# A transformer block on one core: the order of the mixer's groups between the attention heads

## The reference

```
scores = q @ k.T / 8                      # 4 batches x 8 heads, 576 positions, 64 features a head
attn   = softmax(scores, block-causal)    # block of 64
x      = attn @ v                         # heads put side by side: 576 x 512

h = relu(x @ w_in)                        # 512 -> 1024
u, v = h[:, :512], h[:, 512:]
v_n = (v - mean(v)) / sqrt(var(v) + 1e-6)
v_s = w_spatial @ v_n + b_spatial[:, None]  # mixes positions, 576 x 576
x = (u * v_s) @ w_out                     # 512 -> 512

xn  = (x - mean(x)) / sqrt(var(x) + 1e-6) * g_ln
out = x + relu(xn @ w_ch1) @ w_ch2        # 512 -> 2048 -> 512
```

## Time and profile before

| what | us |
|---|---|
| median of three runs | 867.6 |
| lowest, highest | 867.1, 869.02 |
| the profiled execution, time | 869.89 |
| the profiled execution, span from first to last instruction | 868.1 |
| TensorE busy in it | 836.6 (96%) |
| VectorE, ScalarE, GpSimd busy | 348.9, 290.5, 203.2 |
| mean granted clock of TensorE, as a share of full speed | 0.988 |

### The profile page before, as it was taken

One profiled execution on the slowest core, in us unless ns is written; L12 is line 12 of the kernel. 1 busy time (PEld: TensorE's weight loads), 2 busy tenths in 40 slices (PEclk: granted clock), 3 DMA queues, 4 the chain that ended last, 5 costly groups with the idle time before them and its releaser, 6 DMA issues.

```text
span 868.1 us, 13430 instructions
## 1 busy us (share of the span) xinstructions
PE 836.6 (96%) x5064; PEld 709.4 (82%) x5064; DVE 348.9 (40%) x774; ACT 290.5 (33%) x784; POOL 203.2 (23%) x289
## 2 busy tenths in 40 slices
PE   7989999999999999998989999999999999999998
PEld 4766787768877688777969999999999999999997
DVE  5876644365443664417464312213222123122111
ACT  5865654355543554424344111111111111111110
POOL 4874646243341442503341000000000000000000
PEclk9999999999999999999989999999999999999999
DMA  6551321221212221016343003003003002001000
GB/s 212 163 174 42 112 81 42 77 86 58 69 43 76 80 65 42 2 54 194 98 147 114 1 1 109 1 0 109 0 0 109 0 0 90 18 0 43 30 1 36
DMA packets 37681, 56.02 MB, mean 65 GB/s; under 512 B 2749, under 2 KB 20157, under 8 KB 37630
## 3 DMA queue, kind: packets, MB, share of 16 engines
q1 hardware_dynamic: 37630, 55.34, 19.5%
HBM read 45.90 MB, written 9.44 MB: 64 GB/s over the span
## 4 chain that ended last, share of the span: by engine, by line
PE 51%; issue 4%; POOL 1%; DVE 1%; ACT 0%; POOLq 0%; ACTq 0%; DVEq 0%
PE psum L1017 17%; PE psum L1016 17%; PE psum L1015 17%; PE psum L1083 1%; POOL rstd L494 0%; POOL unit_raw L536 0%; DVE mix_buf L820 0%; POOL x_r L503 0%; DVE units_r L864 0%; DVE y_res L921 0%; DVE units_r L866 0%; POOL probs L483 0%; DVE mix_buf L810 0%; ACT x_r L616 0%; ACT units_r L682 0%
## 5 line engine op out<-in xcount | busy, mean ns | idle before, releaser
L908 DVE SCALAR_TENSOR_TENSOR h_r<-psum,h_r 128x384 fp32r<-128x384 f32 x96 | 53.5, 557 | 287.0 <-ACT h_r L709 287.0
L709 ACT ACTIVATE h_r<-psum 128x384 fp32r<-128x384 f32 x96 | 47.2, 492 | 340.5 <-PE psum L1017 340.5
L1015 PE MATMUL psum<-xn_r,units_r 128*128 128x384 f32 x384 | 129.6, 337 | 0.0
L1017 PE MATMUL psum<-xn_r,units_r 128*128 128x384 f32 x384 | 129.3, 337 | 0.0
L1016 PE MATMUL psum<-xn_r,units_r 128*128 128x384 f32 x384 | 128.9, 336 | 0.0
L483 POOL TENSOR_SCALAR probs<-probs,row_inv 128x512 f32<-128x512 f32 (+4 forms) x160 | 95.6, 612 | 139.2 <-DVE row_inv L759 139.2
L569 ACT ACTIVATE probs<-psum,neg_max 128x512 f32<-128x512 f32 (+4 forms) x160 | 89.1, 564 | 95.9 <-DVE neg_max L746 95.7
L746 DVE TENSOR_REDUCE neg_max<-psum 128x1 f32<-128x512 f32 (+4 forms) x160 | 77.6, 535 | 92.5 <-PE psum L938 92.3
L1017 PE MATMUL psum<-units_r,h_r 128*128 128x512 f32 x288 | 113.7, 395 | 0.0
L1016 PE MATMUL psum<-units_r,h_r 128*128 128x512 f32 x288 | 113.5, 394 | 0.0
L1015 PE MATMUL psum<-units_r,h_r 128*128 128x512 f32 x288 | 111.9, 389 | 0.0
(11 more groups left out here) (101 smaller groups left out, 1477.5 us busy)
## 6 DMA issues: line engine op xcount, KB each, us to landing
qk_raw<-qk SPq DMA_DIRECT2D x32, 576.0 KB, 4.0
unit_raw<-w_ch SPq DMA_DIRECT2D x32, 256.0 KB, 3.1
y_norm<-y_scratch SPq DMA_DIRECT2D x6, 768.0 KB, 5.8
y_res<-y_scratch SPq DMA_DIRECT2D x6, 768.0 KB, 4.6
out<-y_res SPq DMA_DIRECT2D x18, 256.0 KB, 2.1
v_raw<-vN SPq DMA_DIRECT2D x16, 256.0 KB, 3.0
y_scratch<-mix_buf SPq DMA_DIRECT2D x16, 256.0 KB, 2.0
w_raw<-w_in SPq DMA_DIRECT2D x8, 256.0 KB, 4.8
```

The lines of the kernel that those rows point to most:

```text
L709: act.activation(h_hi[:, f % HR, :], h_bank[:, f % 2, 0:CHUNK], ACT.Relu).then_inc(h_hi_done, 1)
L908: dve.scalar_tensor_tensor(h_lo[:, f % HR, :], h_bank[:, f % 2, 0:CHUNK], 0.0, h_hi[:, f % HR, :].bitcast(F32), ALU.max, ALU.subtract).the ...
L1015: pe.matmul(dst, a_hi, b_hi, start=start, stop=False)
L1017: return pe.matmul(dst, a_lo, b_hi, start=False, stop=stop)
```

## The change

Six things are done at once.

- `GROUP_STEPS`: the groups of a batch go to the steps of its eight heads as 3, 3, 4, 4, 4, 4, 2, 2, where they went as 3, 3, 3, 4, 3, 3, 3, 4.
- The list is moved by one place (`groups_at`): the first place of a batch's heads now holds w4 of the batch before. The last place after all heads (`groups_at(HEADS, 0)`) is used for w4 of the last batch but one, with its copy and its store.
- The s groups go half by half: d = i % 4, h = i // 4. So w0 waits for the low parts of the first four s groups only, and w2 for all eight.
- ScalarE reads a group at the start of steps 0 and 2 (ahead of the exponentials and copies) and at the end of steps 1 and 3; it did so at the end of every step. `split_at` is three steps after the group, not two; VectorE does the split ahead of the normalisation and the statistics.
- `tail_mixer` is gone. In the tail ScalarE reads u groups ahead of the split of the v group two before, an s group's parts are made in its own turn and ahead of the unit, VectorE does the split of g-2, the normalisation of g-1 and the statistics of g; the store of a w group is issued ahead of the unit loads.
- The transposes of the first chunk come ahead of w3, the `xn_tile` splits after w2.

```diff
-        GROUP_STEPS = [[0, 2, 3], [0, 2, 3], [0, 2, 3], [0, 1, 2, 3], [0, 2, 3], [0, 2, 3], [0, 2, 3], [0, 1, 2, 3]]
+        GROUP_STEPS = [[0, 2, 3], [0, 2, 3], [0, 1, 2, 3], [0, 1, 2, 3], [0, 1, 2, 3], [0, 1, 2, 3], [0, 2], [0, 2]]
-            return [(b, sum(len(r) for r in GROUP_STEPS[:i]) + GROUP_STEPS[i].index(step))]
+            at = GROUPS * b + sum(len(r) for r in GROUP_STEPS[:i]) + GROUP_STEPS[i].index(step) - 1
+            return [(at // GROUPS, at % GROUPS)] if at >= 0 else []
-            return late(n, step, 2)
+            return late(n, step, 3)
...
# SyncE
+            for b, g in groups_at(HEADS, 0):
+                store_y(b, kind_of(g)[1])
...
             for g in range(GROUPS):
+                if kind_of(g)[0] == "w":
+                    store_y(B - 1, kind_of(g)[1])
                 for f in unit_at(g, 2):
                     load_unit(f + US)
-                if kind_of(g)[0] == "w":
-                    store_y(B - 1, kind_of(g)[1])
...
# GpSimd, tail
-                tail_mixer(mixer_read, mixer_finish, g)
+                mixer_read(B - 1, g)
+                if is_kind(g, "s"):
+                    mixer_finish(B - 1, g)
...
# ScalarE
-                    k, d, h = NS * b + i, i // 2, slice(HALF * (i % 2), HALF * (i % 2 + 1))
+                    k, d, h = NS * b + i, i % KD, slice(HALF * (i // KD), HALF * (i // KD + 1))
...
+                    elif i == 0:
+                        act.wait_ge(gate_lo, NS * (b + 1))
                     act.activation(y_stage[0:r, k % 2, :], src[0:r, :], ACT.Copy).then_inc(copied, 1)
...
+                    if step in (0, 2):
+                        for b, g in late(n, step, 1):
+                            mixer_read(b, g)
+                            if kind_of(g)[0] == "s":
+                                mixer_finish(b, g)
...
-                    for b, g in late(n, step, 1):
-                        mixer_read(b, g)
-                        if kind_of(g)[0] == "s":
-                            mixer_finish(b, g)
                     for b, g in split_at(n, step):
                         if kind_of(g)[0] == "v":
                             mixer_finish(b, g)
+                    if step in (1, 3):
+                        for b, g in late(n, step, 1):
+                            mixer_read(b, g)
+                            if kind_of(g)[0] == "s":
+                                mixer_finish(b, g)
...
# ScalarE, tail
-                tail_mixer(mixer_read, mixer_finish, g)
+                if is_kind(g, "u"):
+                    mixer_read(B - 1, g)
+                if is_kind(g - 2, "v"):
+                    mixer_finish(B - 1, g - 2)
+                if not is_kind(g, "u"):
+                    mixer_read(B - 1, g)
+                if is_kind(g, "s"):
+                    mixer_finish(B - 1, g)
...
-                if g == GROUPS - 2:
+                if g == GROUPS - 3:
                     for m in range(CT):
                         xn_tile(0, m, acc_bank)
...
# VectorE
+                    for b, g in split_at(n, step):
+                        mixer_finish(b, g)
                     for b, g in late(n, step, 2):
                         normalise_v(b, g)
                     for b, g in late(n, step, 1):
                         if kind_of(g)[0] != "s":
                             mixer_read(b, g)
-                    for b, g in split_at(n, step):
-                        mixer_finish(b, g)
...
# VectorE, tail
-                tail_mixer(mixer_read, mixer_finish, g, normalise_v)
+                if is_kind(g - 2, "v"):
+                    mixer_finish(B - 1, g - 2)
+                if is_kind(g - 1, "v"):
+                    normalise_v(B - 1, g - 1)
+                mixer_read(B - 1, g)
...
# TensorE
                 else:
                     if i == 0:
+                        pe.wait_ge(gate_lo, NS * b + KD)
+                    elif i == HALF // P:
                         pe.wait_ge(gate_lo, NS * (b + 1))
...
             attend(HEADS - 1)
+            for b, g in groups_at(HEADS, 0):
+                mixer(b, g)
...
-                if g == GROUPS - 1:
+                if g == GROUPS - 2:
                     transpose_xn(0, acc_bank)
                 mixer(B - 1, g)
```

More of the change, by code:

```diff
@@ L311, in bank_free, with is_kind @@
                 eng.wait_ge(copied, NCOPY * b + (g if g < S0 else g - NS) + 1)
-        def tail_mixer(read, finish, g, apply=None):
-            if g and kind_of(g - 1)[0] == "v":
-                read(B - 1, g)
-                finish(B - 1, g - 1)
-            else:
-                if g:
-                    finish(B - 1, g - 1)
-                read(B - 1, g)
-            if apply:
-                apply(B - 1, g)
+        def is_kind(g, kind):
+            return 0 <= g and kind_of(g)[0] == kind
         pieces = []
@@ L627, in mixer_read @@
                         act.wait_ge(vn_lo_done, k - 1)
-                    elif b >= 1 and i == 0:
-                        for s in range(2):
-                            act.wait_ge(y_stored[s], 16 * ((k + 1 - s) // 2))
+                    elif b >= 1:
+                        act.wait_ge(y_stored[k % 2], 16 * (k // 2))
                     act.activation(v_relu[0:r, k % 2, :], src[0:r, :], ACT.Relu).then_inc(copied, 1)
@@ L691, in _ @@
             for g in range(GROUPS):
-                tail_mixer(mixer_read, mixer_finish, g)
+                if is_kind(g, "u"):
[6 more added lines that the diff above has]
+                    mixer_finish(B - 1, g)
                 for f in unit_at(g, 1):
+                    if f == 0:
+                        act.wait_ge(grouped, GROUPS * (B - 1))
                     if f == AFTER_U:
@@ L1041, in mixer @@
                         pe.wait_ge(vn_lo_done, NT * (b + 1))
+                    d, h = i % KD, slice(HALF * (i // KD), HALF * (i // KD + 1))
                     c = slice(P * d, P * (d + 1))
```

## The result

The changed kernel takes 844.8 us (median of 4 runs, 843.9 to 845.2), against 868.3 us for the kernel before beside it (867.1 to 869.8). The ratio is 0.9727, with an interval of 0.9708 to 0.9746: 2.7% faster. The forecast was 845.5. The profiled execution took 844.8 us, its span 843.0 us against 868.1.

What follows compares the result with a forecast made beforehand. TensorE's matmul stream, with its holes and clock, was taken as the bound. Terms 6.0 + 3.3 + 3.1 + 1.6 + 2.4 + 6.3 = 22.7 us off 869.9 gave 847.2, taken as 845.5; range 841.5 to 855.

Steps and rivals of the forecast that it cites:

- 1. w0 behind s7: Heads: half order and the move each remove w0's wait for s7's low part, three times 1.99 us; gain 6.0 us.
- 2. Clock behind them: Heads: without the w0 holes, two falls of the clock to 1.2 GHz behind them go; gain 3.3 us.
- the rival by which they recur without a hole: Clock falls come from something recurring, not these holes, so their gains in heads and tail are lost: 850.5 us, chance 0.05.
- 3. v0 behind x_lo: Heads: v0 moves to step 2, so over 4 us of work covers its wait for x_lo; gain 3.1 us.
- 4. Copies and exponentials: Heads: three small waits for u copies (0.7) and batch 0's hole before first scores (0.85) go; gain 1.6 us.
- 5. The new deal: Heads: dealing groups anew costs 0, with 1.1 us of slack in heads 6 and 7; bounds 0 to 6.6 us.
- The rival counted six thin heads: Holes move into the heads, through late exponentials in heads 6 and 7 and in batch 0: 853 us, chance 0.13.
- 7. Tail, u groups: Tail: copying u0 and u1 first shortens the u groups' holes, clock up; gain 2.4 us, bounds 0.7 to 4.4.
- the rival with a fall in the tail (848.5): The clock falls again behind holes left among the tail's u groups: 848.5 us, chance 0.13.
- 8. Tail, w groups: Tail: s7's end to first hidden tile shrinks from 21.5 to 14.9 us, less 0.3 for a normalised tile; gain 6.3.
- The slower rival (872): ScalarE comes 5.5 us late in each of six thin heads, costing 26.4 us: 872 us, chance 0.03.
- The carry-over to the median: The profiled execution's 2.3 us above the median was taken to carry over mostly, putting 847.2 at 845.5 us.

Runs made afterwards that it cites:

- half_only: The kernel before with only the s groups going half by half, w0 waiting for four low parts and w2 for eight: 856.7 us.
- no_half: The changed kernel with the old order of s groups, w0 waiting for all eight low parts: 854.9 us.
- shift_only: The kernel before with only the group list moved by one place: 871.8 us.
- late6: The changed kernel with six extra ScalarE copies ahead of the exponentials in heads 14, 15, 22 and 23: 855.9 us.
- old_reads: The changed kernel with the old order of ScalarE's reads and VectorE's splits in the heads: 854.2 us.
- old_dealing: The changed kernel with the old deal of groups to heads, 3, 3, 3, 4, 3, 3, 3, 4: 845.2 us.
- units_held: The changed kernel with the tail's first three units after u0, u2 and u4, and GpSimd starting them only behind the last v normalisation: 841.7 us.
- old_tail: The changed kernel with the tail's old orders of reads, splits and stores, and the transposes before w4 again: 851.2 us.
- late2: The changed kernel with two extra ScalarE copies ahead of the exponentials in heads 14, 15, 22 and 23: 845.0 us.
- half_store: The kernel before with the s groups half by half and, in the tail, the store of a w group ahead of SyncE's unit loads: 851.9 us.
- half_transposes: The kernel before with the s groups half by half and the first chunk's transposes and their splits one group earlier in the tail: 852.6 us.

## Why the prediction was right, and where it was not

The time was right within a microsecond, from 22.7 us of terms where the span lost 25.1. Not all of its reasons were.

**1. w0 behind s7 (6.0): the size was right, "taken away twice over" was not.** The holes are gone, and half_only shows that the half order does it. But the move doesn't: no_half has 1.97 us at w0, shift_only 2.46. The step that failed was to count scores, attend and transposes as cover for w0 without asking what they put on ScalarE and GpSimd ahead of s7's parts: exponentials and copies ahead of the high part in shift_only, softmax rows and queries ahead of the low part in no_half.

**2. Clock behind them (3.3): right.** Both falls went with the holes, in half_only and in the changed kernel, where 305 us stand at 1.00. So the rival by which they recur without a hole is out. The rule of thumb of the Trainium skill (TensorE: Matmul & The Clock Gate, "HAM oscillation — how this bites in real kernels") would have kept them, since the gaps that it warns of are longer than these holes. The runs decide against it: other falls stood behind holes of 1.97 us in no_half and 2.18 in late6. That equal holes come with and without a fall, as the prediction took from rows 3, was seen again in both.

**3. v0 behind x_lo (3.1): right.** No wait for it is left, and none came in head 9. The move alone does it: shift_only has none.

**4. Copies and exponentials (1.6): right in size.** No such wait stands between 65.5 and 370.8 us. A second wait for exponentials in batch 0, 0.28 us at 95.77, was not in the part. That the order of reads is what pays for the move I hadn't said: without it the kernel loses 9.3 us (old_reads), at more copies than the three that the part named.

**5. The new deal (0): right**, by old_dealing. The slack was 1.1 us and is 1.1 by late6. The rival counted six thin heads; only four matter, since behind heads 30 and 31 no next scores follow. With the falls late6 lost 11 us for four holes of 2.18, more than the idle time by which I had priced that rival.

**6. Tail, w4 and v (0): right** for w4 and its store. The stretch from v0 to u0 is whole.

**7. Tail, u groups (2.4): the size was 1.4, and a term was wrong.** u0 to u5 took 13.3 us and takes 11.9. I had allowed 0.8 us before u1; it is 1.70. TensorE, ScalarE and VectorE of the changed kernel:

```profile
385.88 0.30 PE L1034 MATMUL psum<-x_r,w_in_r 128*128 128x288 f32 x1
387.88 0.40 PE L1032 MATMUL psum<-x_r,w_in_r 128*128 128x288 f32 x1 [1.70 <-ACT mix_buf L625]
388.12 0.29 PE L1033 MATMUL psum<-x_r,w_in_r 128*128 128x288 f32 x1
388.25 0.29 PE L1034 MATMUL psum<-x_r,w_in_r 128*128 128x288 f32 x1
...
394.62 0.40 PE L1032 MATMUL psum<-x_r,w_in_r 128*128 128x288 f32 x1 [1.70 <-ACT u_buf L629]
```
```profile
387.24 0.59 ACT L625 ACTIVATE mix_buf<-psum 64x512 f32<-64x512 f32 x1 [3.35 <-DVE vn_r L802]
```
```profile
385.62 1.53 DVE L802 TENSOR_TENSOR vn_r<-mix_buf,vn_r 128x512 fp32r<-128x512 f32 x1
...
389.72 2.39 DVE L802 TENSOR_TENSOR vn_r<-mix_buf,vn_r 128x512 fp32r<-128x512 f32 x1 [0.79 <-ACT vn_r L607]
```

v4's copy (387.24) waits for v2's low part, and this took 1.53 us beside a scaling on GpSimd, where alone it takes 0.69. Before u4 the split of v3 takes 2.39 us. The form was as told: ScalarE's unit stands between the split of v4 and the copy of u2, and u4 waits 1.70 us behind it. But it stands later than told, since the split of v3 (389.72) holds up v4's normalisation. The collision was foreseen for the normalisation; that ran alone this time (0.53), and the splits met the scalings. So I had the pair of engines right and the operation wrong, and had priced only one of the two meetings. units_held, which keeps them apart, has neither hole. The rule that the Trainium skill gives (SBUF — State Buffer, "Who interferes with whom"), that a VectorE operation with two SBUF inputs contends with a GpSimd operation that reads SBUF, covers this subtraction; its durations (0.69 alone, 1.53, 2.39 and 4.33 beside scalings) agree. The clock stayed up, so the rival with a fall in the tail (848.5) didn't happen here; in old_tail, with 2.6 us in the same place, it did.

**8. Tail, w groups (6.3): 6.6.** From s7's end to the first hidden tile 21.5 us became 14.85, by these two rows and s7's end at 417.17:

```profile
417.01 0.40 PE L1032 MATMUL psum<-w_out_r,x_r 128*128 128x512 f32 x1
...
432.01 0.34 PE L1032 MATMUL psum<-xn_r,units_r 128*128 128x384 f32 x1
```

The 0.3 us for the third normalised tile did not come. Part 8 didn't say that the half order alone would only have moved the wait: half_only keeps 3.18 of 3.54 us. The store order or the earlier transposes were needed too.

**The term that was missing: what a hole costs beyond its idle time.** The sum was 2.4 us short. In the rows of part 7 the hole at 387.88 has 1.70 us of idle time, but the starts before and behind it lie 2.00 apart where they are usually 0.13 apart, and the next start comes 0.24 later instead of 0.13. That is 1.87 + 0.11 = 1.98 us of lost time: 0.28 more than the idle time. The same sum gives 0.23 us for the hole at 149.84 and 0.26 for that at 176.99 of the kernel before. The change removes eleven holes in the heads, and a whole stretch can be compared, from the first scores at 59.58 to the tail's v0, in the kernel before and in old_dealing, where it has neither a hole nor half speed:

```profile
59.58:387.51 327.93, 316.77 (x2233) 250.16 (x2233) 160.88 (x392) 158.30 (x464) 126.28 (x187) 0.98 0.20 64
58.61:367.67 309.06, 309.06 (x2233) 247.18 (x2233) 163.50 (x394) 160.45 (x465) 124.05 (x187) 1.00 0.21 68
```

327.93 less 11.0 us of holes and 5.0 for half speed (1.7 in the opening, 3.3 in the heads) is 311.9: 2.8 us more than 309.06, for eleven holes 0.25 each. So the shortfall lies in the heads. Without the opening's half speed they gave 17.5 us, (327.9 - 1.7) - (311.7 - 3.0), where parts 1 to 5 had 14.0; the tail gave 8.4 where parts 7 and 8 had 8.7; and the opening took 0.8 back.

**The carry-over to the median.** I took 845.5 where the profiled execution's sum gave 847.2, for its being 2.3 us above the median. After the change the profiled execution stands at the median (844.8), so nothing of that difference carried over. The choice took off 1.7 us for a reason that did not hold, and this made up for most of the 2.4 us that the sum lacked: the closeness of 845.5 to 844.8 is in part luck. The opening's clock belongs to it: 3.4 us at half speed in the profile of before, 6.8 after, and none in that of old_dealing, an execution of 841.7 us where that kernel's median is 845.2. Nothing that the change touches lies there, so single executions differ by 3 us for this.

**The slower rival (872)** needs ScalarE 5.5 us late in heads 6 and 7; nothing of the kind is in the trace, and late2 shows that even 1.1 us more costs nothing.

**What stays open.** Why one hole has a fall behind it and an equal one has none is not known. The half order with the tail's new orders, but without the move and the new reads, wasn't tried as one kernel. The nearest is half_store (851.9), which lacks the tail's new order of copies too: move, reads, deal and that order are worth 7.1 us together on top of it. What the half order, the reads, the deal and the tail's orders are worth is known as what each costs when it alone is undone; the move was never undone alone, and the tail's orders only all at once.

## What to carry to other kernels

Before counting work that is moved in between as cover, list what that work itself puts on the engines that make the awaited operand: here the move alone (871.8 us) gave one wait for another, and paid only together with an order that makes the operand earlier (half by half) and reads it first. When a wait is removed in front of a chain, look in the same trace for the next one behind it, here a store queued behind loads on SyncE, and price a hole with its fall of the clock and its restart, not by its idle time. Two operations that hold each other up, as VectorE's subtraction and GpSimd's scaling, are best kept apart by a wait on constants: that gave 3.1 us more than the change.

## What the runs showed of the hardware

- A fall to 1.2 GHz stood behind some of the equal holes and not behind others: one of two of 1.97 us (no_half) and two of four of 2.18 us (late6). The hole of 2.6 us among the tail's u groups stands in six kernels; three profiled executions have a fall behind it (before, half_store, old_tail), three have none (half_only, half_transposes, shift_only). None was seen behind the holes of 1.55 to 1.75 us.
- A hole cost TensorE 0.2 to 0.3 us more than its idle time: 0.23, 0.26 and 0.28 us from the starts around three holes, and 0.25 in the mean of eleven.
- A subtraction of 128x512 on VectorE took 0.69 us alone, 1.53 beside one scaling on GpSimd, 2.39 beside two, and 4.33 beside four in a row: it waited through the whole row, not for one instruction.
- The same opening was at half speed for 0, 3.4 or 6.8 us in different executions, with nothing changed in it.
